# Soft-MoE block on one core: the low parts of x at a batch's end, and a third place for the MLP's weights in the staging memory

## What is computed

```python
# q, k, v: (4, 8, 576, 64); f: (4, 8, 576)
scores = q @ k.T / sqrt(64) + cum[:, None] - cum[None, :]      # cum = cumsum(log(clip(f)))
attn = softmax(causal(scores)) @ v                             # x = attn, heads side by side: (2304, 512)
h = x @ w_in                                                   # w_in (512, 2048)
x2 = (h * sigmoid(1.702 * h)) @ w_out                          # w_out (2048, 512)
logits = x2 @ phi                                              # 32 slots, 4 for each of 8 experts
slot_input = softmax(logits, tokens).T @ x2
slot_out[e] = relu(slot_input[e] @ w1[e]) @ w2[e]              # w1 (512, 1024), w2 (1024, 512)
out = softmax(logits, slots) @ slot_out
```

## Time and profile before

| What | Before |
|---|---|
| median of 3 runs | 751.52 us (751.29 to 754.44) |
| profiled execution, its own time | 751.85 us |
| its span | 749.9 us |
| TensorE busy | 702.9 us (94%) |
| VectorE, ScalarE, GpSimd busy | 439.7, 443.2, 438.8 us |
| mean granted clock | 0.992 |
| MLP's matmuls (L1261) in the chain that ended last | 48% of the span |
| HBM read, written | 103.03 MB, 4.79 MB |

### The profile page before, as it was taken

The page is one execution under the profiler, slowest core; times in us unless marked ns, Lnnn a source line. Parts: engine busy times, 40 slices in busy tenths (PEclk is TensorE's granted clock), DMA queues, the critical chain, the costliest instruction groups (busy, mean ns, idle before and its releaser), DMA issues.

```text
span 749.9 us, 15808 instructions
## 1 busy us (share of the span) xinstructions
PE 702.9 (94%) x5923; PEld 666.8 (89%) x5923; DVE 439.7 (59%) x1223; ACT 443.2 (59%) x1063; POOL 438.8 (59%) x511
## 2 busy tenths in 40 slices
PE   3999999999999899999999999999999999998993
PEld 3888889999999899999999899999999999995662
DVE  6788867776776556676655566766542432224423
ACT  4788976576758576676675675757555344311113
POOL 3355668585858766777777685958476476520000
PEclk9999999999999999999999999999999999999997
DMA  4433544545545353364544525453224354599976
GB/s 106 108 94 108 140 104 124 124 104 123 116 123 124 101 121 112 108 138 118 131 115 82 133 88 117 127 133 103 62 62 137 127 187 152 158 404 363 385 293 252
DMA packets 102650, 108.84 MB, mean 145 GB/s; under 512 B 62832, under 2 KB 72048, under 8 KB 100528
## 3 DMA queue, kind: packets, MB, share of 16 engines
q1 hardware_dynamic: 102576, 107.85, 49.8%
HBM read 103.03 MB, written 4.79 MB: 144 GB/s over the span
## 4 chain that ended last, share of the span: by engine, by line
PE 74%; DVE 8%; ACT 8%; issue 4%; POOL 3%; DMA 1%; SPq 0%; DVEq 0%; POOLq 0%
PE mb L1261 48%; PE yb L1112 6%; PE zb L1132 5%; PE xb L1158 5%; PE mb L1313 2%; ACT prob L733 2%; PE xb L1092 2%; DVE prob L889 2%; PE yb L1352 1%; DVE ptl L895 1%; POOL xl L677 1%; DMA stage<-in_moe_w_in 1%; PE mb L1081 1%; ACT gate L783 1%; ACT pth L749 1%
## 5 line engine op out<-in xcount | busy, mean ns | idle before, releaser
L1261 PE MATMUL mb<-xh,wih 128*128 128x288 f32 x512 | 157.6, 308 | 8.3 <-DVE hid L976 4.2
L1261 PE MATMUL mb<-gh,woh 128*128 128x288 f32 x512 | 156.4, 305 | 3.9 <-DVE x2t L983 3.7
L1261 PE MATMUL mb<-gl,woh 128*128 128x288 f32 x512 | 150.8, 294 | 0.0
L1261 PE MATMUL mb<-gh,wol 128*128 128x288 f32 x512 | 150.8, 294 | 0.0
L1261 PE MATMUL mb<-xh,wil 128*128 128x288 f32 x512 | 150.8, 294 | 0.0
L1261 PE MATMUL mb<-xl,wih 128*128 128x288 f32 x512 | 150.7, 294 | 0.0
L687 POOL TENSOR_TENSOR gl<-hid,gh 128x288 fp32r<-128x288 f32 x128 | 103.6, 815 | 35.9 <-ACT gh L777 35.2
L976 DVE SCALAR_TENSOR_TENSOR hid<-gate,mb 128x288 f32<-128x288 f32 x128 | 57.6, 450 | 107.6 <-ACT gate L783 107.2
L733 ACT ACTIVATE prob<-prob,m_row 64x576 f32<-64x576 f32 (+4 forms) x160 | 96.4, 604 | 34.6 <-DVE m_row L877 33.6
L704 POOL TENSOR_TENSOR wil<-stage,wih 128x512 fp32r<-128x512 f32 x64 | 81.9, 1289 | 48.7 <-ACT wih L719 46.3
L704 POOL TENSOR_TENSOR wol<-stage,woh 128x512 fp32r<-128x512 f32 x64 | 82.7, 1292 | 45.2 <-ACT woh L719 45.1
(11 more groups left out here) (201 smaller groups left out, 1470.7 us busy)
## 6 DMA issues: line engine op xcount, KB each, us to landing
stage<-in_moe_w_in SPq DMA_DIRECT2D x64, 256.0 KB, 3.8
stage<-in_moe_w_out SPq DMA_DIRECT2D x64, 256.0 KB, 2.7
ring_a<-in_moe_w SPq DMA_DIRECT2D x16, 1024.0 KB, 6.8
ring_b<-in_moe_w SPq DMA_DIRECT2D x14, 1024.0 KB, 12.5
qk_in<-in_q SPq DMA_DIRECT2D x32, 144.0 KB, 2.9
qk_in<-in_k SPq DMA_DIRECT2D x32, 144.0 KB, 3.1
v_in<-in_v SPq DMA_DIRECT2D x32, 128.0 KB, 3.0
result<-ring_a SPq DMA_DIRECT2D x16, 256.0 KB, 3.0
```

What stands on the lines that cost most here:

```text
L1261: ins = mm(bank[:, 0:HALF], a[:, t, P * (j % 4):P * (j % 4) + P], x[:, t, cols], start=(i == 0), stop=(i == 11))
```

## The change

It has three parts.

1. In `batch_steps`, at slot 8 of batches 1 and 2 (where a further batch follows), GpSimd's three low parts of x stand one by one behind units 56, 57 and 58 rather than together before unit 56. VectorE's low part of piece 3 stands behind unit 58 rather than before unit 57. At slot 8 of batch 3 the order stays as it was, and so does ScalarE's everywhere.
2. `stage` gets a third place. A piece goes to place `order % 3`, its transfer waits for the low part of the piece three before it, and there are three semaphores for arrivals.
3. To make room, `gap` goes, `woh` and all behind it moves up by 256 floats, and `ew` moves into the memory of the tail's second half, `tail_b`.

```diff
@@ -66,6 +66,7 @@
+STAGES = 3
@@ -232,8 +233,13 @@
             steps += (f() + vsplit + pt(0) + (late if engine == "dve" else []) + f() + score(1) + pt(1) + f() + score(2) + pt(2)
-                      + qk + f() + score(3) + pt(3) + dup + f() + norm + f() + early
-                      + (early_x + f() + pv + xs[3] if s == 0 else f()) + f(2))
+                      + qk + f() + score(3) + pt(3) + dup + f() + norm + f() + early)
+            if s == 0 and following and engine == "pool":
+                steps += f() + xs[0] + f() + xs[1] + f() + xs[2]
+            elif s == 0 and following and engine == "dve":
+                steps += f() + pv + f(2) + xs[3]
+            else:
+                steps += (early_x + f() + pv + xs[3] if s == 0 else f()) + f(2)
@@ -281,10 +287,9 @@
-        stage = sb("stage", [P, 2, QF], F32, mlp_mem)
+        stage = sb("stage", [P, STAGES, QF], F32, mlp_mem)
...
-        sb("gap", [P, 256], F32, mlp_mem)
@@ -325,7 +330,6 @@
-        ew = sb("ew", [P, BATCH * QT, SLOTS], F32, tail_a)
@@ -344,6 +348,7 @@
+        ew = sb("ew", [P, BATCH * QT, SLOTS], F32, tail_b)
@@ -382,7 +387,7 @@
-        w_dma = [sem(f"w_dma{i}") for i in range(2)]
+        w_dma = [sem(f"w_dma{i}") for i in range(STAGES)]
@@ -507,8 +512,8 @@
-                slot = t % 2
-                wait_from(sp, w_lo, order - 1)
+                slot = order % STAGES
+                wait_from(sp, w_lo, order - STAGES + 1)
@@ -701,7 +706,7 @@
-                pool.tensor_tensor(lo[:, t, :], stage[:, t % 2, :], hi[:, t, :].bitcast(F32),
+                pool.tensor_tensor(lo[:, t, :], stage[:, order % STAGES, :], hi[:, t, :].bitcast(F32),
@@ -715,8 +720,8 @@
-                act.wait_ge(w_dma[t % 2], 16 * ((order >> 1) + 1) if isinstance(order, int) else (order - t % 2) * 8 + 16)
-                nc.scalar.copy(hi[:, t, :], stage[:, t % 2, :]).then_inc(w_hi, 1)
+                act.wait_ge(w_dma[order % STAGES], 16 * (order // STAGES + 1))
+                nc.scalar.copy(hi[:, t, :], stage[:, order % STAGES, :]).then_inc(w_hi, 1)
```

## The result

The changed kernel takes **745.07 us** at the median (744.44 to 745.34, 6 runs) against 751.44 of the kernel before on the same chip (751.27 to 754.44, 6 runs). The ratio is 0.9906, with a 95% interval of 0.9891 to 0.9922. That is 6.4 us less, where 6.3 was forecast. The profiled execution took 745.00 us, and its span is 743.1.

A forecast was written before the change was run, and what follows sets the result against it. TensorE was taken as the bound, with four stalls at two batch ends to remove. Gains of 3.15 and 3.73 less a loss of 0.6 gave 6.3 us, so a median of 745.2 us, range 743.2 to 748.3.

The forecast's parts named there:

- four stalls: TensorE waits for `x2t` before units 59 and 0 at the ends of batches 1 and 2, in sum 6.9 us.
- 0.27 for each restart: Cost added to the idle time of each of TensorE's stalls at the ends of batches 1 and 2.
- Gain: 1.58 + 1.57 = 3.15: Stalls before unit 59 at the ends of batches 1 and 2 go through VectorE's new order: 3.15 us.
- The margins of 0.7 and 1.0: Before unit 0 at a batch's end, `x2t` is ready 0.7 us early and the fourth `wil` 1.0.
- 3.73: Gain in us from GpSimd's order and the third place: stalls before unit 0 go at both ends, 1.79 + 1.94.
- The loss of 0.6: Normalisation behind unit 0 touches GpSimd's work on `kh` and `kl`: 0.3 us charged at each of two ends.
- The sum of 6.3: Total gain forecast for the whole kernel: 3.15 + 3.73 - 0.6 = 6.3 us.
- B: Normalisation falls under GpSimd at both ends, costing 3.0 instead of 0.6: gain 3.9 us, 747.6; chance 0.08.
- C: GpSimd's low parts run into inner heads' normalisations in batches 2 and 3: 4.9 us slower, 756.4; chance 0.04.
- D: Always-early weights also remove some of TensorE's waits for `hid`: gain 8.3 us, 743.2; chance 0.08.

The follow-up runs named there:

- the last run: The change plus earlier GpSimd masks in batch 1's heads (before both unit groups at the first) and the new order at batch 3's end: 741.80 us, ratio 0.9855.
- D+G: VectorE's and GpSimd's new orders on the kernel before, still with two staging places: 746.23 us, ratio 0.9912.
- S: The third staging place alone on the kernel before, both orders as before: 750.10 us, ratio 0.9966.
- D+S: VectorE's new order and the third staging place on the kernel before, GpSimd's order as before: 749.01 us (one run).
- the run of D: VectorE's new order alone on the kernel before, GpSimd's order and two staging places as before: 754.23 us, ratio 1.0020.

## Why the prediction was right

**Where the time is.** Right: TensorE is the bound, and four stalls are all that the change can reach. 6.9 was said, 6.87 is measured between the first MLP matmul and unit 0 of batch 2. The idle times plus 0.27 for each restart were a good price for these four. It is not a general one: the stalls that went in batch 1's stage gave back only 0.1 to 0.2 more than their idle times (3.89 for 3.41 in the last run).

**VectorE's part.** The times came as worked out. In the clock of the run before, 0.55 later than here, units 57 and 58 start to leave at 245.3. But the step "Gain: 1.58 + 1.57 = 3.15" for VectorE's part is right only with GpSimd's part beside it. Alone it is worth nothing, since `gl` for unit 60 was 0.54 us from being late. The end of `gl` stood in the earlier trace rows and the start of unit 60 in the trace, and the prediction did not compare them.

**GpSimd and the third place.** Unit 0 was forecast at 257.0, and starts at 256.42 + 0.55 = 257.0. `x2t` of unit 62 was forecast at 256.3 and is out at 255.54 + 0.46 + 0.55 = 256.55. The fourth `wil`, forecast at 256.0, is done at 253.70 + 1.29 + 0.55 = 255.5. The margins of 0.7 and 1.0 came out at 0.4 and 1.5. The first is the one that counts, and D+G, with 0.26 of waiting there, shows how thin it is. What the text left open is who pays: of 3.73 the third place carries 0.6 in the presence of both orders. It could have been worked out, since with two places piece 3 lands some 3 us earlier by the two orders alone.

**The loss of 0.6.** This term was wrong. The normalisation behind unit 0 takes 1.27 us (257.90), as it does alone, because `kl` on GpSimd was done by 257.35. So the charge stood for nothing. The two engines did meet 12 us earlier, in `xl` and `wil`, at 0.5 us each. Nothing was late for it: behind them VectorE still stood 1.09 us for TensorE before the result at 249.44, and the fourth `wil` was 1.5 us early.

**From the trace to the median.** The sum of 6.3 met the median's 6.4 by two things that nearly cancel, which is luck: the charge that was not due, and about 0.5 us of scatter. The profiled executions differ by 6.85 us (751.85 and 745.00), but the one before stood 0.41 above its median of 6 runs and the one after 0.07 below. Within the 6.85 a start 0.5 us earlier and a tail 0.8 us longer, neither of which is the change's work (the same kernel profiled again started 0.4 later than the one before, and its tail was as long), also nearly cancel. In another set of runs the same kernel was 7.4 us ahead.

**Rivals B, C and D.** None came about in the change. No normalisation between 262 and 530 us is over 2.5 us long, and TensorE's waits for `hid` are the same 4.2 us in six places before and after, to the place. With the new orders the third place is without effect in the interior, in both directions. With GpSimd's old order it is not: in S and in D+S it went with a new wait at unit 2 behind an end, through a late piece of `woh` and ScalarE's queue, at 0.5 and 0.8 us. No rival had that path.

## What to carry to other kernels

When an engine that bounds the kernel stands twice in a row, look at what would be late if the first stall went, before giving each stall a price: here the parts were worth -1.8, 2.4 and 2.7 us singly and 6.9 together, and the two orders alone 6.3. Read for each release how long before its use it came, not only those that came too late. And where one engine holds up the other's instructions, look for the point at which its queue stops anyway, as GpSimd's does at the masks, and put that point ahead of the work that it would hold up.

## What the runs showed of the hardware

**GpSimd can hold up a VectorE instruction for as long as its queue runs without a pause.** The normalisation of four instructions takes 1.27 us with GpSimd idle, 1.34 beside the end of one GpSimd instruction, 3.35 beside three and up to 4.18. The traces show where the time goes. In the kernel before, VectorE's first instruction of such a four, and GpSimd beside it:

```profile
203.98 3.20 DVE L889 TENSOR_SCALAR prob<-prob,rsum 128x128 f32<-128x128 f32 x1
```

```profile
203.78 0.80 POOL L687 TENSOR_TENSOR gl<-hid,gh 128x288 fp32r<-128x288 f32 x1
204.55 2.54 POOL L704 TENSOR_TENSOR wil<-stage,wih 128x512 fp32r<-128x512 f32 x2
```

The first of the four takes 3.20 us and not 0.29, and ends at 207.18, 0.1 behind the last of GpSimd's three. The other three take 0.34, 0.41 and 0.47, as they do alone, and GpSimd's take their usual 0.8 and 1.3. Six more normalisations between 113 and 241 us in this trace begin with such a first instruction, and each of these ends 0.1 us behind GpSimd's run: the one at 113.89 takes 2.37, where GpSimd runs until 116.18, the one at 131.22 takes 1.94, where it runs until 133.07. So in this kernel the price of a normalisation under GpSimd is the length of GpSimd's unbroken run behind its start. That is why the masks, at which GpSimd waits for VectorE, shorten it when they stand earlier: at 114.40 in the last run the first of the four takes 0.35.

The Trainium skill, SBUF — State Buffer, section "Who interferes with whom", says that issue order decides which of the two blocks, and for the whole instruction. The traces agree that VectorE is blocked outright and not slowed. They show more than the section says, since at 203.98 VectorE stays blocked not for the one GpSimd instruction that was running (until 204.58) but for the two behind it too.

By the same section a VectorE instruction with two inputs in this memory contends with a GpSimd instruction that reads it. `xl` shows that: 0.76 us in batch 0 with GpSimd idle, 0.9 to 1.1 beside two `xl` of GpSimd, and 1.54 to 1.70 beside `xl` and `wil`. Here GpSimd pays as well: its `wil` took 1.82 us and not 1.3.

**The granted clock fell once behind a few microseconds of standing.** In the run of D it went to 0.50 behind waits of 0.96 and 1.78 us that lay 9 us apart, and that cost 1.56 us. The same kernel's second end, with 0.95 and 2.33, kept it. So a change that moves waiting about without removing it can lose time that no wait shows. One event does not show what brings the drop about. Nor do such drops explain all of the wide scatter of the kernel before (750.3 to 754.8 us, where the change has 744.4 to 745.3): its three executions with a mean clock of 0.985 or less took 753.8 to 754.8, but those at 0.991 to 0.993 spread from 750.7 to 754.0.
